# One level of Strassen's identity in the up products of two feed-forward stages

## What is computed

```python
# q, k, v: 2 x 8 heads x 768 x 64
scores = np.where(q_bucket == k_bucket, scale * q @ k.T, -1e9)
x = softmax(scores) @ v                     # then 1536 tokens x 512
h = x @ w_in                                # 512 x 2048
x = (h - np.tanh(h)) @ w_out                # 2048 x 512
for e in range(4):                          # second stage
    h = np.maximum(x @ w1[e], 0.0)          # 512 x 1024
    out += p[:, e:e + 1] * (h @ w2[e])      # 1024 x 512
```

## Time and profile before

| | us |
|---|---|
| median of 3 runs | 1066.65 (1065.93 to 1067.14) |
| the profiled execution | 1066.52 |
| its span, first to last instruction | 1064.7 |
| TensorE (PE) busy | 1040.6 (98%) |
| VectorE (DVE) busy | 487.9 (46%) |
| ScalarE (ACT) busy | 359.1 (34%) |
| GpSimd (POOL) busy | 262.5 (25%) |

### The profile page before, as it was taken

How to read it: one execution, slowest core, us unless ns; L and a number is a source line. 1 busy time by engine, 2 the same in 40 slices (tenths; PEclk the granted TensorE clock), 3 DMA queues, 4 the chain that set the end, 5 groups by cost and what they waited for, 6 DMA issues and landing times.

```text
span 1064.7 us, 15679 instructions
## 1 busy us (share of the span) xinstructions
PE 1040.6 (98%) x5726; PEld 967.1 (91%) x5726; DVE 487.9 (46%) x822; ACT 359.1 (34%) x680; POOL 262.5 (25%) x305
## 2 busy tenths in 40 slices
PE   7999999998999999999999999999999999999998
PEld 5988988888999999999989899898998989989897
DVE  6878877887343333333543333333333333333322
ACT  4778777775322322223411121111212112121110
POOL 3698878877222312223100000000000000000000
PEclk9999999999999999999999999999999999999999
DMA  4544554443201011010110101101011010100011
GB/s 127 135 127 126 133 133 126 128 135 89 97 23 41 20 40 34 27 41 20 40 40 20 40 21 40 39 20 39 20 39 37 22 39 20 39 0 0 0 59 59
DMA packets 28721, 59.52 MB, mean 56 GB/s; under 512 B 3760, under 2 KB 5904, under 8 KB 28688
## 3 DMA queue, kind: packets, MB, share of 16 engines
q1 hardware_dynamic: 28528, 58.68, 18.9%
q10 hardware_dynamic: 160, 0.39, 0.1%
HBM read 44.07 MB, written 3.19 MB: 44 GB/s over the span
## 4 chain that ended last, share of the span: by engine, by line
PE 91%; POOL 4%; DVE 3%; issue 1%; ACT 1%; DMA 0%; POOLq 0%; ACTq 0%; SPq 0%
PE ps L1011 38%; PE ps L1028 25%; PE ps L1040 13%; PE ps L923 5%; PE ps L953 4%; PE ps L934 4%; PE ps L897 2%; DVE pT_lo L697 1%; POOL k_st L420 1%; POOL q_lo L407 1%; DVE prob L690 0%; POOL k_st L414 0%; POOL x_f L452 0%; POOL x_lo L469 0%; DMA proj_raw<-in_proj 0%
## 5 line engine op out<-in xcount | busy, mean ns | idle before, releaser
L1011 PE MATMUL ps<-x_hi,w_lo 128*128 128x384 f32 x768 | 258.1, 336 | 1.3 <-issue 1.3
L1011 PE MATMUL ps<-x_hi,w_hi 128*128 128x384 f32 x768 | 258.0, 336 | 0.0
L1011 PE MATMUL ps<-x_lo,w_hi 128*128 128x384 f32 x768 | 257.9, 336 | 0.0
L636 ACT ACTIVATE g_hi<-ps 128x384 fp32r<-128x384 f32 x128 | 63.0, 492 | 433.5 <-PE ps L1011 433.5
L853 DVE SCALAR_TENSOR_TENSOR g_lo<-ps,g_hi 128x384 fp32r<-128x384 f32 x128 | 71.3, 557 | 203.1 <-ACT g_hi L636 203.1
L1028 PE MATMUL ps<-w_hi,g_hi 128*128 128x512 f32 x384 | 150.4, 392 | 0.0
L1028 PE MATMUL ps<-w_lo,g_hi 128*128 128x512 f32 x384 | 150.3, 392 | 0.0
L1028 PE MATMUL ps<-w_hi,g_lo 128*128 128x512 f32 x384 | 150.3, 392 | 0.0
L1011 PEld LDWEIGHTS ps<-x_hi,w_lo 128*128 128x128 f32 x768 | 144.0, 188 | 2.8 <-issue 1.5
L1011 PEld LDWEIGHTS ps<-x_lo,w_hi 128*128 128x128 f32 x768 | 144.1, 188 | 1.3
L1011 PEld LDWEIGHTS ps<-x_hi,w_hi 128*128 128x128 f32 x768 | 144.0, 188 | 0.0
(11 more groups left out here) (102 smaller groups left out, 1427.4 us busy)
## 6 DMA issues: line engine op xcount, KB each, us to landing
w_raw<-in_w SPq DMA_DIRECT2D x32, 512.0 KB, 3.7
q_raw<-in_qT SPq DMA_DIRECT2D x32, 192.0 KB, 3.3
k_raw<-in_kT SPq DMA_DIRECT2D x30, 192.0 KB, 3.3
w_raw<-in_w_in SPq DMA_DIRECT2D x8, 512.0 KB, 4.1
w_raw<-in_w_out SPq DMA_DIRECT2D x8, 512.0 KB, 4.5
v_raw<-in_vP SPq DMA_DIRECT2D x16, 192.0 KB, 2.8
inv_rows<-inv_dram SPq DMA_DIRECT2D x16, 192.0 KB, 3.3
k_hi<-k_st SPq DMA_DIRECT2D x15, 192.0 KB, 3.5
```

The source lines that it names most:

```text
L636: act.activation(g_hi[:, f, :], up_ps[:, f, 0:CHUNK], ACT.Relu).then_inc(g_hi_ready, 1)
L1011: mm = pe.matmul(up_ps[:, f, 0:CHUNK], w, x, start=k + m == 0, stop=k == KT - 1 and m == 2)
```

## The change

The four 256 x 256 quadrants of x and the quadrants of a weight group are combined in Winograd's form of Strassen's identity. A group has now G = 256 hidden columns (8 groups in stage one, 16 in stage two) and is split in two by hidden tile and two by depth; x is split by depth and by token half (384). A block (i, r) is a group (2i + r % 2) against 768 tokens (r // 2): seven block products of 2 x 3 matmuls in place of eight. The products are accumulated in four banks (`u_ps`, two in turn by block, `v_ps` and `z_ps`), the down tiles in the other four; what two sums share is copied out by ScalarE (`take_c1`, `take_c2`, `take_c5`) and added by VectorE (`add_parts`). TensorE weaves the down tiles of the block before between the products. The weight sums are made by GpSimd (`up_sums`), rounded by ScalarE (`up_round`, `down_round`), completed by GpSimd (`up_rest`) and VectorE (`down_rest`). The x sums and their split are made in the attention (first 768 tokens, in pairs 5, 6 and 7, counted from 0), after it (the others), and between the stages. `x_round` and `x_rest` of each pair go.

```diff
-            engine.dma_start(w_raw[:, 2 * c:2 * c + 2, :],
-                             rows.rearrange("(t p) n -> p t n", p=P)).then_inc(w_loaded[c], 16)
+        def load_up(engine, cols):
+
+            for slot, j, f in ((0, 0, 0), (1, 1, 0), (7, 0, 1), (2, 1, 1)):
+                rows = cols[2 * j * P:2 * (j + 1) * P, f * P:(f + 1) * P]
+                engine.dma_start(wu_raw[:, slot, :, :],
+                                 rows.rearrange("(k p) n -> p k n", p=P)).then_inc(wu_loaded, 16)
...
+                def load(group, up, down):
+                    sp.wait_ge(wu_lo_ready, group)
+                    load_up(sp, up)
+                    sp.wait_ge(wd_lo_ready, group)
+                    load_down(sp, down)
...
+                def up_sums(group):
+
+                    pool.wait_ge(wu_loaded, 64 * group + 64)
+                    pool.tensor_tensor(wu_raw[:, 3, :, :], wu_raw[:, 7, :, :], wu_raw[:, 2, :, :],
+                                       ALU.add).then_inc(w_sum1, 1)
+                    pool.tensor_tensor(wu_raw[:, 5, :, :], wu_raw[:, 0, :, :], wu_raw[:, 7, :, :], ALU.subtract)
+                    pool.wait_ge(w_sum1, 2 * group + 1)
+                    pool.tensor_tensor(wu_raw[:, 4, :, :], wu_raw[:, 3, :, :], wu_raw[:, 0, :, :],
+                                       ALU.subtract).then_inc(w_sum1, 1)
+                    pool.wait_ge(w_sum1, 2 * group + 2)
+                    pool.tensor_tensor(wu_raw[:, 6, :, :], wu_raw[:, 1, :, :], wu_raw[:, 4, :, :],
+                                       ALU.subtract).then_inc(w_sums, 1)
...
+                def stage1(i, r):
+                    if not (isinstance(i, int) and i + r == 0):
+                        pi, pr, _ = earlier(i, r, False, 1)
+                        hidden_rest(pi, pr, 3, 1, 0, 3)
+                    if r == 0:
+                        up_sums(2 * i + 1)
+                    hidden_rest(i, r, 0, 0, 0, 0)
+                    if r in (0, 3):
+                        if isinstance(i, int) and i + r == 0:
+                            pool.wait_ge(o_full, 2 * HEADS)
+                        up_rest(2 * i + 1 if r == 0 else 2 * i + 2, 1 if r == 0 else 0, 0)
+                    hidden_rest(i, r, 1, 0, 1, 1)
+                    if r in (0, 3):
+                        up_rest(2 * i + 1 if r == 0 else 2 * i + 2, 1 if r == 0 else 0, 1)
+                    hidden_rest(i, r, 2, 1, 1, 2)
+                    if r == 2:
+                        up_sums(2 * i + 2)
...
+                    hidden_round(i, r, 0, 0, 0, 0)
+                    if start:
+                        up_round(1, 1)
+                    if r == 0 and not start:
+                        act.wait_ge(sum21_full, count_of(i, 0))
+                        up_round(2 * i + 1, 1)
+                        down_round(2 * i, 0)
+                    if r == 1:
+                        down_round(2 * i + 1, 1)
+                    take_c2(i, r, False)
...
+                    def first():
+                        dve.wait_ge(sum11_full, n + 1)
+                        dve.wait_ge(c1_ready, n + 1)
+                        dve.tensor_tensor(hb[:, 0, :], v_ps, hb[:, 0, :], ALU.add).then_inc(h11_ready, 1)
...
+                def split_x(c):
+                    for slot in (3, 4, 6):
+                        x_sum(c, slot)
+                    for slot in DVE_REST:
+                        x_rest(c, slot)
+
+                for r in range(4):
+                    stage1(I1 - 1, r)
+                split_x(2)
+                stage2(I1, 0, 0, 0, after1=True)
+                split_x(3)
...
-                def up(par, c, tiles=range(FC)):
+                def product(par, b, wslot, xslot, to, start):
+
+                    (wh, wl), (xh, xl, _) = wu[par], xq[b]
+                    for k in range(2):
+                        for m, (w, x) in enumerate(((wl, xh), (wh, xl), (wh, xh))):
+                            mm = pe.matmul(to, w[:, wslot, k, :], x[:, xslot, k, :],
+                                           start=start and k + m == 0, stop=k == 1 and m == 2, skip_group_check=not start)
+                    return mm
...
+                    need(xlo_dve, 4, 1)
+                    product(par, b, 0, 0, u, True).then_inc(u1_full, 1)
+                    wait(pe, h11_ready, n)
+                    need(xlo_dve, 4, 2)
+                    product(par, b, 1, 1, v_ps, True).then_inc(sum11_full, 1)
+                    if between:
+                        between()
+                    down(0)
+                    wait(pe, h12_ready, n)
+                    need(xlo_dve, 4, 3)
+                    product(par, b, 3, 3, z_ps, True).then_inc(z5_full, 1)
+                    down(1)
+                    pe.wait_ge(c1_ready, n + 1)
+                    need(xlo_dve, 4, 4)
+                    product(par, b, 4, 4, u, False).then_inc(u6_full, 1)
+                    pe.wait_ge(c5_ready, n + 1)
+                    need(xlo_pool, 3, 1)
+                    product(par, b, 6, 2, z_ps, False).then_inc(sum12_full, 1)
+                    down(*((2, 3) if psecond else (2, 3, 4)))
+                    pe.wait_ge(c2_ready, n + 1)
+                    need(xlo_pool, 3, 2)
+                    product(par, b, 5, 5, u, False).then_inc(sum22_full, 1)
+                    down(*((4, 5) if psecond else (5, 6, 7)))
+                    pe.wait_ge(h22_ready, n + 1)
+                    need(xlo_pool, 3, 3)
+                    product(par, b, 2, 6, u, False).then_inc(sum21_full, 1)
...
+                place_block(0, 0, False, call=0, between=finish_attention)
+                pe.wait_ge(last_summed, 2)
+                place_block(0, 1, False)
+                place_block(0, 2, False, call=1)
```

More of the change, by code:

```diff
@@ L364, in _ @@
[L364 to L370 removed]
+                    for q in range(GE):
+                        hidden = slice(q * G, (q + 1) * G)
+                        load(G1 + GE * e + q, w1[e][:, hidden], w2[e][hidden, :])
@@ L498, in pair @@
                                 x_add(it - 1, 0)
-                            if later and b == 1:
-                                x_round(it - 1)
-                                x_rest(it - 1)
                         if qt == 3 and not last:
@@ new lines, in split_x, with stage2 @@
+                def split_x(c):
+                    x_sum(c)
+                    for slot in POOL_REST:
+                        x_rest(c, slot)
+                def stage2(i, r, more=True):
+                    if r == 0:
+                        up_sums(2 * i + 1)
+                    if r in (0, 3) and (more or r == 0):
+                        for part in range(2):
+                            up_rest(2 * i + 1 if r == 0 else 2 * i + 2, 1 if r == 0 else 0, part)
+                    if r == 2 and more:
+                        up_sums(2 * i + 2)
@@ L533, in _ @@
+                with pool.Fori(I1 + 1, I2 - 1) as i:
+                    for r in range(4):
+                        stage2(i, r)
+                stage2(I2 - 1, 0, more=False)
             @block.scalar
@@ L655, in _ @@
+                stage2(I1, 0, begins=True)
+                for slot in HI_ORDER:
+                    x_round(3, slot)
+                for r in range(1, 4):
+                    stage2(I1, r)
+                with act.Fori(I1 + 1, I2 - 1) as i:
+                    for r in range(4):
+                        stage2(i, r)
+                for r in range(4):
+                    stage2(I2 - 1, r, more=False)
+                positive(I2 - 1, 3, 3, 1, 0, 3, (sum21_full, count_of(I2 - 1, 4)))
             @block.vector
@@ new lines, in _ @@
+                stage1(0, 0)
+                x_sum(1, 3)
+                x_rest(1, 0)
+                stage1(0, 1)
+                last_scale(0)
+                last_scale(1)
+                x_sum(1, 4)
+                x_sum(1, 6)
+                for slot in DVE_REST[1:]:
+                    x_rest(1, slot)
+                stage1(0, 2)
+                stage1(0, 3)
+                with dve.Fori(1, I1 - 1) as i:
+                    for r in range(4):
+                        stage1(i, r)
```

870 lines of the change are left out of this document (559 added, 311 removed).

## The result

| | before | after |
|---|---|---|
| median | 1066.89 us (4 runs, 1065.93 to 1067.39) | 1056.81 us (4 runs, 1056.25 to 1058.94) |
| ratio, 95% interval | | 0.991 (0.9893 to 0.9927) |
| the profiled execution, its span | 1066.52, 1064.7 | 1058.94, 1056.9 |

The account below looks back on a forecast made before the run. TensorE, busy 98% of the span, was taken as the bound. From 1066.5: -50.0 (removed matmuls), +4.5 (steady block), +23.5 (seams), -4.4 (attention) gave 1040.1, forecast as 1040 us; range 1018 to 1062.

Parts of the forecast that it names:

- the seams: Four places in the feed-forward part where cover for late engines is missing: +23.5 us in sum (12 to 32).
- the port: VectorE operations with two SBUF inputs are held up by GpSimd operations; without this the sum would be about 14 us lower.
- (3): Between the stages, both token halves are split in a lump behind the block's own work: 5.4 to 10.6, taken as 8.5 us.
- (4): Second lump ahead of block (I1,1) holds ScalarE 6 and VectorE 7 us; P5's copy late by 2, with port 3.0 us.
- The steady block: Feed-forward blocks of 15.6 us (stage one) and 15.7 (stage two), with weight-trip waits and spill: +4.5 us (0 to 20).
- (c): Rival: weight round trip outlasts its four blocks, stalling each of 11 trips 2.5 us more: 1067, no change; chance 0.11.
- (d): Rival: VectorE's third sum, held by the shared port, comes late for P7 in every block: 1088 at 1.0 us; chance 0.09.
- (e): Rival: products are not fewer, or the split costs what it saves in matmuls: 1090 us; chance 0.03.
- (1): Block (0,0), with no down tiles ahead: waits at P6, P7 and the next block, 1.3 + 0.8 + 2.9 = 5.0 us.
- (2): Tokens 768 to 1535 split only after the last head; P2 of (0,2) waits 4.6 to 6.4, in all taken as 7.0 us.
- Rival (b): TensorE's clock falls to its lower level at the long gaps of three seams: 3 x 1.65 = +5, 1045 us; chance 0.14.
- The attention: GpSimd loses x_round and x_rest, ending stalls in pairs 1 to 4; queueing in late pairs costs: -4.4 us (-13 to +3).

Follow-up runs that it names:

- the last version: The kernel with all three x splits spread between block operations, plus two more edits of order at blocks (I1,0) and (0,1): 1035.42 us, ratio 0.9697.
- the run with the second split alone: Changed kernel with only the x split in block (0,1) spread between its operations, last_scale and GpSimd's first-block up remainders moved ahead: 1050.29 us, ratio 0.9837.

## Why the prediction was wrong in size

Against the profiled execution the sum was 1040.1, measured 1058.9; the 18.8 us by its own terms (against the median, 1056.81, it is 16.7). Two steps failed: the price of the lumps at the seams, which left the port almost out of seams (3) and (4), and the clock, which was left out of the sum.

- **The removed matmuls, -50.0: right to about 1.0.** The steady block of stage two is 15.68 us for 15.7, and taking five more matmuls away took 0.91 us a block. In stage one, 360 matmuls between two trips take 63.72 us where 62.5 was forecast: 0.73 of the 1.22 is the wait at the trip, a late first matmul of P7 makes 0.1, and the rest is 1 ns a matmul.
- **The steady block, +4.5: 2.3 too dear.** The trips cost 3 x 0.73 by the starts, near their 0.8, and stage two nothing. P7 never waited in a steady block, so rivals (c), (d) and (e) fall. `hidden_sub` rose to 663 ns in the mean and `positive_rest` to 699 where they read two SBUF tiles, the port as forecast, without effect behind the cover that the blocks have.
- **The seams, +23.5: 30.5 of idle time measured.** (1) came as forecast in all three of its waits: 1.19, 1.14 and 2.57 for 1.3, 0.8 and 2.9 (for the last the prediction's own 14.4 - 11.7 gives 2.7). (2) is 7.4 for 7.0, all of it at P2, which had 4.6 to 6.4. The term that was mis-sized is (4), 9.0 for 3.0. The step reads: the lump "holds ScalarE 6 us and VectorE 7 us; P5's copy comes 2 us late, 3.0 with the port". The port was given 1.0 us there; it added 13.7 - 8.1 = 5.6 us to VectorE's lump, and behind it stand the first sum of the block, ScalarE's relu of it, and only then the copy that P5 wants. With most of the port's share gone the idle time is still 3.6, where the prediction had 2 without the port; with the lump taken apart it is 0.2.
- **Seam (3), 8.5 for 8.5, is luck.** The prediction had VectorE's three `x_sum` and first `x_rest` take 4.0 us, 5.2 with the port, so 3.7 to 4.9 of wait at P1, and the rest at P2 and at a late copy for P6. Measured, nearly all of it stands at P1 (8.24, then 0.24 at P2, nothing at P6), since those four operations took 8.6 us:

```profile
519.60 1.19 DVE L989 TENSOR_TENSOR xq_raw<-acc 128x768 f32<-128x768 f32 x1
520.82 4.95 DVE L989 TENSOR_TENSOR xq_raw<-acc,xq_raw 128x768 f32<-128x768 f32 x2
525.69 5.05 DVE L1001 TENSOR_TENSOR xq_lo<-acc,xq_hi 128x768 fp32r<-128x768 f32 x2
```

So the prediction had used the alternation (each operation behind one of GpSimd) for seam (2) and forgot it for (3) and (4). The late copy for P6 is real too: it came out, as 4.10 us, when the lump was spread.
- **The clock, left out of the sum: 9.8 us of matmul time.** Rival (b) named it and gave it 3 x 1.65 = 5. Its mechanism was right; that 4.4 us of the time hang on it by the run that fills the gaps is close to the 5 by luck, since the loss is 1.9 to 2.9 a seam, four times, and about half of it reached the end. Three seams were to lose 5 us and more by the prediction's own working; with them in the sum, the clock belonged there too. The prediction also says that before has no gap above 2 us to test it. It has one, just ahead of the low clock from which the 1.65 was taken (row and window of before):

```profile
13.46 0.72 PE L923 MATMUL ps<-k_hi,q_lo 128*128 128x512 f32 x1 [2.14 <-DVE k_hi L756]
...
13.00:17.00 4.00, 3.54 (x11) 2.80 (x12) 2.02 (x4) 2.20 (x4) 3.19 (x4) 0.57 0.14 39
```

The Trainium skill, TensorE: Matmul & The Clock Gate, section "The HAM clock gate (the "warmup" mystery)", says that an idle TensorE drops to half rate; this trace agrees (0.53 of full clock, 320 ns against 173.6).
- **The attention, -4.4: 4.2 measured**, as the part begins at 253.77 for 257.98; the agreement is in part luck. The four waits of pairs 1 to 4 are gone (7.8 us; undoing it cost 6.2), the 1.27 at the end too, and the idle time between 170 and 250 us, in the last pairs, rose from 4.5 to 7.6, less than the 4.7 charged. That makes -6.0. Against it stands a low clock in pair 5 (counted from 0) that costs 1.6 us of matmul time and that the prediction did not have. In the run with most of GpSimd's part taken away, which has no low clock in that pair, the part begins at 252.68. That the rise in the last pairs comes from the split's operations is not shown; no run took them away.
- **The port** was priced at about 14 us of the sum. The part of it that was tested, two lumps, gave 8.9. The Trainium skill, SBUF — State Buffer, section "SBUF: two separate sides", states a lock for the whole instruction; the fall to 0.95 agrees, and the pairs at 2.5 us agree to 0.3, as whole instructions one after another would take 2.8.

So 18.8 = 7.0 of idle time at the seams + 9.8 of clock + 3.7 that the brackets leave out + 1.0 of rest - 3.1 (three trips at 0.46 for 4.5) + 0.4 in the attention and at the ends. The runs with less clock loss or less port show that these parts are not independent: what one wait gives back the next takes in part, so the order in which they are named decides the split.

## What to carry to other kernels

When a change takes work off the engine that bounds, walk the places where its cover is missing (the first block, the turn between stages) in queue order: a lump of 7 operations that nobody wants yet, ahead of a copy that is wanted now, cost 10 us here, and one by one between the block's own operations they cost 0.2. Two engines that share a port are one queue for operations between SBUF tiles: count their times as a sum (2.5 us a pair here, 2.8 one after the other), and see whether giving all to one, or moving them apart in time, is shorter. If a sum has TensorE idle for some microseconds at a stretch, put the slower clock behind it into the sum too.

## What was not expected of the hardware

In the lumps VectorE and GpSimd run in step at 2.5 us an operation each, and the quicker engine suffers most: 0.95 us becomes 2.5, 1.85 becomes 2.5.

The clock also fell where no single standstill was longer than 2.57 us (261 to 275: gaps of 1.19, 1.14 and 2.57, a loss of 2.6), and in the last version behind one of 2.46 (a loss of 1.7), but not at the 1.94 us stalls of the attention before, where it stays at 1.00. The length of the standstill alone does not decide it, and executions differ. In the attention of the changed kernel it fell behind one of 1.59; the same stall in the run with the second split alone left it at 1.00 (a row and a window of the changed kernel, then the same window of that run):

```profile
177.60 0.33 PE L1326 MATMUL ps<-ident,prob 128*128 128x128 f32 x1 [1.59 <-DVE pT_lo L955]
...
176.00:184.00 8.00, 6.41 (x32) 6.05 (x32) 6.23 (x9) 4.84 (x10) 6.32 (x7) 0.79 0.42 110
...
176.00:184.00 8.00, 7.00 (x42) 6.14 (x43) 7.88 (x13) 5.40 (x12) 5.59 (x7) 1.00 0.46 123
```

So a single profile can hold a low clock that the kernel does not always have, and a few us of a difference between two of them can be that. How it is decided was not tried.
